# Attention stage of a one-core MoE kernel: q loaded in rows of six tokens, outputs computed in two row halves of the array

## What is computed

```
kv = np.einsum('bhsd,bhse->bhde', k, v)
out = np.einsum('bhsd,bhde->bhse', q, kv)
rms = np.sqrt(np.mean(out * out, axis=-1, keepdims=True) + 1e-06)
return (out / rms * g_norm).astype(np.float32)
```

## Time and profile before

| | |
|---|---|
| median of 3 runs | 1157.27 us (1157.14 to 1159.4) |
| the profiled execution, its own time | 1156.55 us |
| its span | 1155.0 us |
| PE busy | 1127.1 us, 98% of the span |
| DVE, ACT, POOL busy | 732.2, 454.6, 657.8 us |
| attention stage on PE | to 72.37 us |

### The profile page before, as it was taken

How to read it: one execution, slowest core, us unless ns; L and a number is a source line. 1 busy time by engine, 2 the same in 40 slices (tenths; PEclk the granted TensorE clock), 3 DMA queues, 4 the chain that set the end, 5 groups by cost and what they waited for, 6 DMA issues and landing times.

```text
span 1155.0 us, 18656 instructions
## 1 busy us (share of the span) xinstructions
PE 1127.1 (98%) x6184; PEld 993.1 (86%) x6185; DVE 732.2 (63%) x1160; ACT 454.6 (39%) x807; POOL 657.8 (57%) x609
## 2 busy tenths in 40 slices
PE   8989999999999999999999999999999999999996
PEld 7878999988989888988989888988987888888885
DVE  3876888888875878888875878888662222222221
ACT  4774444444534444444534444444322222222220
POOL 1477777799867777799867768777330111111101
PEclk8999999999999999999999999999989999999998
DMA  9936877777712348777712348777379849427960
GB/s 236 248 88 207 283 281 273 278 258 267 254 37 73 113 154 299 273 263 266 256 37 73 112 156 300 271 260 279 137 265 355 308 182 360 162 93 300 364 252 13
DMA packets 102434, 250.87 MB, mean 217 GB/s; under 512 B 8255, under 2 KB 48191, under 8 KB 94172
## 3 DMA queue, kind: packets, MB, share of 16 engines
q1 hardware_dynamic: 97360, 235.18, 59.3%
q0 software_dynamic: 4800, 14.72, 3.6%
q10 hardware_dynamic: 203, 0.05, 0.0%
HBM read 170.99 MB, written 79.98 MB: 217 GB/s over the span
## 4 chain that ended last, share of the span: by engine, by line
PE 85%; DVE 6%; POOL 3%; issue 2%; DMA 2%; ACT 1%; SPq 0%; DVEq 0%; POOLq 0%; ACTq 0%
PE ps L1257 27%; PE ps L1259 26%; PE ps L1258 26%; PE ps L1446 2%; PE ps L1350 1%; PE ps L1214 1%; PE ps L1412 1%; DVE hT_lo L941 1%; DVE x_rows L952 1%; DMA w_raw<-in_moe_w_dram 1%; DVE hT_lo L934 1%; PE ps L1335 1%; DMA q<-in_q_dram 1%; DVE hT_lo L939 1%; POOL x_ops_lo L515 1%
## 5 line engine op out<-in xcount | busy, mean ns | idle before, releaser
L1257 PE MATMUL ps<-x_ops_hi,w_hi 128*128 128x384 f32 x672 | 226.9, 338 | 4.1 <-DVE sum L922 4.0
L1257 PE MATMUL ps<-w_hi,hT_hi 128*128 128x512 f32 x576 | 227.3, 395 | 1.8 <-DVE x_rows L952 1.5
L1259 PE MATMUL ps<-x_ops_hi,w_lo 128*128 128x384 f32 x672 | 225.8, 336 | 0.0
L1259 PE MATMUL ps<-w_hi,hT_lo 128*128 128x512 f32 x576 | 225.3, 391 | 0.0
L1258 PE MATMUL ps<-w_lo,hT_hi 128*128 128x512 f32 x576 | 225.1, 391 | 0.0
L1258 PE MATMUL ps<-x_ops_lo,w_hi 128*128 128x384 f32 x672 | 225.0, 335 | 0.0
L952 DVE SCALAR_TENSOR_TENSOR x_rows<-ps,dense_probs,x_rows 128x512 f32<-128x512 f32 x270 | 190.2, 738 | 22.9 <-PE ps L1259 22.9
L607 POOL DMA_INDIRECT out_dram<-y_rows,row_ids x22 | 22.6, 1027 | 236.2 <-DVE y_rows L1155 141.8
L491 POOL TENSOR_TENSOR w_lo<-w_raw,w_hi 128x512 fp32r<-128x512 f32 x96 | 148.4, 1566 | 8.0 <-ACT w_hi L694 8.0
L1145 DVE TENSOR_TENSOR rhT_lo<-ps,rhT_hi 128x512 fp32r<-128x512 f32 x44 | 28.4, 686 | 172.0 <-ACT rhT_hi L813 172.0
L477 POOL TENSOR_TENSOR w_lo<-w_raw,w_hi 128x512 fp32r<-128x512 f32 x48 | 62.3, 1299 | 129.9 <-ACT w_hi L684 129.9
(11 more groups left out here) (198 smaller groups left out, 2013.3 us busy)
## 6 DMA issues: line engine op xcount, KB each, us to landing
w_slots<-split_parts SPq DMA_DIRECT2D x64, 1024.0 KB, 5.8
w_raw<-in_moe_w_dram SPq DMA_DIRECT2D x96, 512.0 KB, 3.6
ahead_raw<-in_moe_w_dram SPq DMA_DIRECT2D x64, 512.0 KB, 6.7
split_parts<-ahead_hi SPq DMA_DIRECT2D x64, 512.0 KB, 3.9
split_parts<-ahead_lo SPq DMA_DIRECT2D x64, 512.0 KB, 5.7
row_tile<-dispatched_rows POOLq DMA_DIRECT2D x20, 257.0 KB, 5.4
kv<-in_k_dram SPq DMA_DIRECT2D x16, 288.0 KB, 8.0
kv<-in_v_dram SPq DMA_DIRECT2D x16, 288.0 KB, 8.9
```

What stands on the lines that cost most here:

```text
L1257: mm(out_, ah, bh, start=(first and m == 0), stop=False, skip_group_check=not final or not first)
L1259: last = mm(out_, al, bh, start=False, stop=(final and m == n - 1), skip_group_check=not final or not first)
```

## The change

- q is loaded by one DMA per unit, laid out as k and v are: six following tokens on a partition, runs of 6 x 64 floats. The six transposes stay six; each now takes tokens 2j and 2j+1 of the six.
- `kv_blocks` holds for each head the 64x64 block once on partitions 0 to 63 and once on 64 to 127, 64 columns wide, with no zeros. ACT writes it alone: one copy of 128x64 for the halves that stay where they are, and two of 64x64 for those that cross. `copy_kv` on DVE and the zeroing on POOL go.
- `outputs(u)` has 12 matmuls rather than six: even tokens with weights and data on rows 0 to 63, odd tokens on rows 64 to 127, 64 columns moving, the two going to two PSUM banks (`out_banks`).
- PE runs 8 filler matmuls at the start of `products_in(1)` and 3 between its k-v products and its transposes.
- The x parts on ACT are made in turns 5, 7, 10, 11, 12, 13, 14 rather than 5, 7, 10, 11, 11, 12, 12.

```diff
-    QG = S // (2 * NP_)
+    QG = SJ // 2
...
-    qs = [at(f"q{s}", [NP_, QG, 2, 2 * DH], F32, (o if s < 2 else kvq23) + 9216 * (s % 2) + 6144) for s in range(KVS)]
+    qs = [at(f"q{s}", [NP_, 2, KHD], F32, (o if s < 2 else kvq23) + 9216 * (s % 2) + 6144) for s in range(KVS)]
...
-                for h in range(2):
-                    sp.dma_start(qs[s][:, :, h, :], q_h[u, h]).then_inc(q_in[s], 16)
+                sp.dma_start(qs[s][:, :, :], q_u[u]).then_inc(q_in[s], 16)
...
-            g.memset(kvb[:, :, :, :], 0.0).then_inc(consts_made, 1)
...
                 A(qT[:, s, :, :], qT_banks, ACT.Copy).then_inc(in_copied, 1)
+                A(kvb[:, s, 0, :], psf[:, KV0:KV0 + DH], ACT.Copy).then_inc(in_copied, 1)
                 for h in range(2):
-                    hp = slice(h * DH, (h + 1) * DH)
-                    A(kvb[hp, s, h, hp], psf[hp, KV0:KV0 + DH], ACT.Copy).then_inc(in_copied, 1)
+                    A(kvb[(1 - h) * DH:(2 - h) * DH, s, 1, :], psf[h * DH:(h + 1) * DH, KV0:KV0 + DH], ACT.Copy).then_inc(in_copied, 1)
...
-                for i, at_ in zip(X_ORDER, (5, 7, 10, 11, 11, 12, 12)):
+                for i, at_ in zip(X_ORDER, (5, 7, 10, 11, 12, 13, 14)):
...
-            def copy_kv(u, s):
-
-                dve.wait_ge(in_copied, 3 * u + 3)
-                if u == 0:
-                    dve.wait_ge(consts_made, 1)
-                for h in range(2):
-                    hp, other = slice(h * DH, (h + 1) * DH), slice((1 - h) * DH, (2 - h) * DH)
-                    V.tensor_copy(kvb[other, s, h, other], psf[hp, KV0:KV0 + DH]).then_inc(kv_copied, 1)
...
+            def fillers(n):
+                for _ in range(n):
+                    mm(ps[:, 7, 0:P], ident[:, :], ident[:, :], start=True, stop=True)
+
             def products_in(u, s, n_in):
 
+                if u == 1:
+                    fillers(2 * WARM // 3)
                 if u:
-                    pe.wait_ge(in_copied, 3 * u)
-                    pe.wait_ge(kv_copied, 2 * u)
+                    pe.wait_ge(in_copied, 4 * u)
...
+                if u == 1:
+                    fillers(WARM // 4)
+                pe.wait_ge(q_in[s], n_in // 2)
...
-                        to = out_bank[s][:, j * 2 * P:(j + 1) * 2 * P].rearrange("p (t h d) -> p t h d", t=2, h=2)[:, :, h, :]
-                        last = mm(to, qT[:, s, h, j * NP_:(j + 1) * NP_], kvb[:, s, h, :].rearrange("m (t d) -> m t d", t=2), start=True, stop=True)
+                        for t in range(2):
+                            tp = slice(t * DH, (t + 1) * DH)
+                            last = mm(out_banks[s][:, t, (2 * j + h) * DH:(2 * j + h + 1) * DH], qT[tp, s, h, j * NP_:(j + 1) * NP_],
+                                      kvb[tp, s, h if t == 0 else 1 - h, :], start=True, stop=True)
```

More of the change, by code:

```diff
@@ L113, in build @@
     qT = at("qT", [P, 2, 2, QH], F32, o2)
-    kvb = at("kv_blocks", [P, 2, 2, P], F32, o2 + 4608)
-    sq = at("squares", [NP_, QW], F32, o2 + 6656)
+    kvb = at("kv_blocks", [P, 2, 2, DH], F32, o2 + 4608)
+    sq = at("squares", [NP_, 2, QW // 2], F32, o2 + 6656)
     hsum = at("head_sums", [NP_, 3, 4 * QG], F32, o2 + 9728)
@@ L242, in seq @@
                 "u two (p j) d -> u p two (j d)", p=NP_)
-        k_u, v_u = seq(k), seq(v)
-        q_h = q.rearrange("b (u two) s d -> (b u) two s d", two=2).rearrange("u two (g p t) d -> u two p g (t d)", t=2, p=NP_)
+        q_u, k_u, v_u = seq(q), seq(k), seq(v)
         w1a_u = w1a.rearrange("e (c p) (f n) -> e f p c n", p=P, n=FQ)
@@ L252, in build @@
         qT_banks = psf[:, 0:1024].rearrange("m (h n) -> m h n", h=2)[:, :, 0:QH]
-        out_bank = [psf[0:NP_, (2 + 2 * s) * 512:(2 + 2 * s) * 512 + QW] for s in range(2)]
-        xT_bank = psf[:, 6 * 512:6 * 512 + QW].rearrange("m (g t p) -> m g p t", t=2, p=P)[:, :, 0:NP_, :]
+        out_banks = [ps[0:NP_, 2 + 2 * s:4 + 2 * s, 0:QW // 2] for s in range(2)]
+        xT_bank = psf[:, 6 * 512:6 * 512 + QW].rearrange("m (j p) -> m j p", p=P)[:, :, 0:NP_].rearrange("m j (g p) -> m g p j", g=SPB)
         KV0 = 512 + 320
@@ L449, in _ @@
             g.memset(fill[:, :], 0.0).then_inc(consts_made, 1)
-            pool.wait_ge(consts_made, 7)
+            pool.wait_ge(consts_made, 6)
             pool.wait_ge(powers_made, 2)
@@ L655, in square @@
                 act.wait_ge(o_done, u + 1)
-                A(sq[:, :], out_bank[s], ACT.Square).then_inc(o_squared, 1)
+                A(sq[:, :, :], out_banks[s], ACT.Square).then_inc(o_squared, 1)
             def root(u):
@@ L967, in _ @@
             dve.wait_ge(p_step, 7)
-            dve.wait_ge(consts_made, 14)
+            dve.wait_ge(consts_made, 13)
             steps = [0]
@@ L1223, in transposed @@
                     pe.wait_ge(x_out, u)
-                for j in range(2 * QG):
-                    last = tr(psf[:, 6 * 512 + j * P:6 * 512 + j * P + NP_], yn[:, s, j * P:(j + 1) * P], ident[0:NP_, 0:NP_])
+                for t in range(2):
+                    for j in range(QG):
+                        to, of = 6 * 512 + (2 * j + t) * P, (t * QG + j) * P
+                        last = tr(psf[:, to:to + NP_], yn[:, s, of:of + P], ident[0:NP_, 0:NP_])
                 last.then_inc(xT_done, 1)
-            pe.wait_ge(consts_made, 3)
-            for _ in range(WARM):
-                mm(ps[:, 7, 0:P], ident[:, :], ident[:, :], start=True, stop=True)
+            pe.wait_ge(consts_made, 2)
+            fillers(WARM)
             products_in(0, 0, 32)
```

25 lines of the change are left out of this document (10 added, 15 removed).

## The result

The changed kernel takes 1183.55 us (median of 4 runs, 1180.21 to 1184.87), the kernel before 1157.2 (1156.11 to 1159.4) beside it on the same chip: a ratio of 1.023, with a 95% interval of 1.0213 to 1.0247. The forecast was 1149.3, with 1154.7 as the high end. The profiled execution took 1183.71, its span is 1182.0 against 1155.0.

What follows compares the result with a forecast made beforehand. PE, busy 98% of the span, bounds the kernel; in attention the loop and loads are near-bounds. Terms -5.0 - 2.2 - 0.3 - 0.5 = -8.0 against 1156.55, with the median 0.7 above that execution: 1149.3 us, range 1147.5 to 1154.7.

Steps and rivals of the forecast that it cites:

- Rival 1: Attention loop: the clock falls to 1.2 GHz, 2.2 us per unit; half the units gives 1162 us; chance 8%.
- rival 3: Ramp: the clock falls there all the same, -3 in place of -5.0, 1151.3 us; chance 12%.
- The ramp, -5.0: Start of attention stage: fillers keep the clock up, so outputs 3 start at 22.35 rather than 27.37.
- Outputs, 0.87 us: A unit's 24 row-half output records take 0.87 us rather than 1.40; bounds 0.80 and 1.78.
- rival 4: Outputs: weight loads of the row halves run alone, outputs 1.78 us, 1158.3 us in all; chance 9%.
- The loop, 6.66: Two-unit attention loop: 7.03 + 0.16 (ACT) - 0.53 (outputs) = 6.66 us; six loops give -2.2.
- X parts, -0.3: Twelve units of the loop: spreading ACT's doubled x parts over turns saves 0.3 us (0 to 0.7).
- the end, -0.5: Outputs 15, ahead of the dense stage, are 0.53 us shorter.
- The pace of 2.8: Attention-stage loads: q's longer rows bring a unit's loads from 3.51 to 2.8 us, no longer a bound.
- Rival 2: Attention-stage loads keep their pace of 3.5 us a unit; gain at most 2.7, 1154.6 us; chance 9%.
- unit 4 there near 19: End of ramp: loads at 2.8 us a unit bring unit 4 near 19 us; it is needed at 19.5.
- a dense stage that hands the gain back: Sign of being wrong: the dense stage's first steps wait for POOL and hand the 8 us back.

Runs made afterwards that it cites:

- the kernel with fillers in units 6 to 8: Changed kernel plus three whole-array filler matmuls ahead of the outputs of units 6, 7 and 8 only: 1166.65 and 1168.78 us.
- the whole-array kernel: Changed kernel's q load, fillers and moved x parts, but outputs, kv_blocks and copies as in the kernel before: 1156.73 us, ratio 1.000.
- the changed kernel with 128 columns: Changed kernel with each row-half output matmul reading its 64 columns twice, so 128 stream: 1158.82 us, ratio 1.0032.
- one filler: Changed kernel plus one whole-array filler ahead of every unit's outputs: two executions at 1157.23 and 1159.12 us, seven from 1184.29 to 1192.03, one at 1170.07.
- the kernel with fillers in units 0 to 5: Changed kernel plus three whole-array filler matmuls ahead of the outputs of units 0 to 5 and none after: 1165.78 us.

## Why the prediction was wrong, step by step

**The step that failed** is the one that left the clock full in the loop. Rival 1 named the mechanism, with 8% and, for its price, half of the units. It held in all of them, after a fall in the ramp (rival 3's condition). The argument against it, PE busy for 1.70 of 3 us at clock 1.00, was taken from a loop whose outputs stream 128 columns, and I carried it over to a loop of 64-column records. The change had altered just what the row's evidence rested on. Nor did I ask the two questions apart: what lets a full clock fall, and what brings a fallen one back. In the kernel before, the fall in the ramp cost 10 us of half clock because the loop with outputs of 128 columns restored it; with 64 a like fall costs the whole stage.

**Its price.** 2 x 2.76 = 5.5 us for a unit at 1.2 GHz was nearly right: 5.70. What was mis-sized is how long it lasts: 2.2 for each of twelve units is 26.4, and with the -8.0 that makes 1175.7. Counted on the traces, the forecast's first dense matmul at 64.37 became 96.51: 5.45 of the 32.1 between are the ramp (27.80 for 22.35), 25.3 the twelve units (66.60 for 41.27) and 1.4 the end (2.11 for 0.73). The half clock at the start of the dense stage costs some 2 more, which makes 34.1 of the 34.25 from 1149.3 to 1183.55.

**The ramp, -5.0.** Measured +0.43. Its first part held: fillers under other waits, clock 1.00 to 15.08, outputs 0 at 13.17 (forecast 12.85; a wait of 0.58 for probs_rows had been left out). Rival 3, the clock falling in the ramp all the same, thus happened, but was priced on the loop's recovering from it. The term was too large even with the clock held: the kernel with fillers in units 6 to 8 runs the changed kernel's own program up to unit 5, and in its execution the clock stayed full to 27.06. Its outputs 3 start at 23.91, 3.5 us earlier than before. Of the missing 1.5, 1.1 is outputs 0 at 13.92 for 12.85, and the rest the three units.

**Outputs, 0.87 us.** 1.16 at full clock in the changed kernel itself (13.17 to 14.33), 1.17 in others. Within the bounds of 0.80 and 1.78, and the halves do overlap (rival 4 is out). The size was off because I took a pair of 96-column weight loads for the k-v pair's 72 ns: it is 1.17 / 12 = 97, where k-v pairs with 64 weight columns have 0.85 / 12 = 71. The Trainium skill, page TensorE: Matmul & The Clock Gate, section LDWEIGHTS, has a weight load go by its columns at 1.2 a nanosecond; 80 ns for 96 and 53 for 64 differ by 27, and the measured pairs by 26. I had set the rule aside for the transposes' row, and for sizes between two widths it was the better guide.

**The loop, 6.66.** 6.94 where the clock was held. ACT's +0.16 was +0.06 (1.73 for 1.83), the outputs' -0.53 was -0.23, and a third term, put at nothing, is +0.10: row-half outputs start 0.62 us behind the transposes ahead of them (58.42 to 59.04 in the kernel with fillers in units 6 to 8), where it was 0.52 (33.88 to 34.40 in the earlier trace rows). The three make it 6.96. So -0.5 for six loops rather than -2.2.

**X parts, -0.3, and the end, -0.5.** The first was not measured apart; the whole-array kernel, with the spread x parts and a full clock, takes 44.45 for the twelve units where it was 43.77, so no gain is seen (an "issue" pause of 1.12 us is in it). The end was +0.88 at half clock; at full clock 1.40 to 1.17 would be -0.2. PE waited for nothing of POOL at the start of the dense stage.

**Loads.** SP's long waits came as forecast. The pace of 2.8 didn't: 3.2 to 3.35. At half clock that cost nothing. Where the clock held it did, right behind the ramp: PE waits for the k-v load of unit 5 for 1.65 us with fillers in units 6 to 8 and for 1.55 in the changed kernel with 128 columns (27.09). Rival 2 was the better guess on the pace, and the forecast's "unit 4 there near 19" left no room for it. Later in the stage nothing waits for loads.

**Had the clock held,** the terms as measured would be -3.5, -0.5 and -0.2, but the wait for the load takes back part of the first at once. The k-v products of unit 5 start at 26.80 in the kernel with fillers in units 6 to 8, and in the kernel before here:

```profile
28.78 0.92 PE L1199 MATMUL ps<-kv 96*64 96x64 f32 x24
```

That is 2.0 us, so some 2.7 in all at the first dense matmul, an estimate from these rows. In the whole-array kernel 2.1 there became a ratio of 1.000 (0.9987 to 1.0014) at the end. The forecast named a dense stage that hands the gain back among what would make it wrong, without a price. Nor do the chances of its list add up to the 0.80 for faster: 0.58, 0.12 and half of 0.09 are 0.75. So no version run here beats the kernel before; those that hold the clock end 0.0 to 0.4% from it.

**Open.** What tips the clock isn't settled. Of the nine traced executions with fillers in unit 1, two lost it near 15 us: those with the longest wait for probs_rows near 12 us, 0.58 (the changed kernel) and 0.82 (one filler). The seven others waited for 0 to 0.51 there and held it past that point; 0.50 is that of the kernel with fillers in units 6 to 8, whose program is the same up to unit 5. That sorts the traces, and a load that comes a little sooner or later may be why one program holds the clock in some executions and loses it in others, but no run has varied this wait alone. Later, pauses of 1.3 to 2.2 us stood ahead of the falls in loops of 64-column records, while one of 1.55 did nothing in the changed kernel with 128 columns, nor did this one in the kernel before (clock 1.00 in 69 to 72):

```profile
70.62 0.69 PE L1225 MATMUL ps<-ident,attn_rows 96*128 96x96 f32 x6 [1.30 <-DVE x_raw L880]
```

Two of these pauses are "issue", in which PE waited for nothing that the profile names. The longest, in the kernel with fillers in units 0 to 5, and its DMA queue of instructions from 46 to 55 us:

```profile
51.13 0.45 PE L1189 MATMUL ps<-kv 96*64 96x64 f32 x8 [2.22 <-issue]
```

```profile
q8 instruction: 1, 0.02, 0.9%
```

That one packet has 16 KB, from 48.51 to 49.78, while PE stands from 48.91 on. Each of the four "issue" pauses over 0.7 us in these traces ends 1.3 to 1.7 us behind such a packet (35.59 behind 33.94, 51.93 behind 50.22, 35.58 behind 33.99), and the packets come further apart where PE is slower: 8 to 9 us in the kernel before from 41 us on, 12 to 14 in the changed kernel from 43 on. So PE may have waited for its own instructions, with the queues full of loads; that isn't tested.

## What to carry to other kernels

When a change makes matmuls smaller, the clock at which they run is part of its price: a row that shows PE at full clock at a low busy share speaks only for the matmuls in that row, and "busy 100%" at clock 0.50 may be a state that the loop never leaves. Ask separately what the new loop does with a full clock and what it does with a fallen one, and look for pauses ahead of a fall (0.58 to 2.2 us here). A gain in a stage is a gain only if what the next stage waits for (here the load of w_raw and POOL's sums) comes earlier too, and if the loads can follow: here outputs 3 came 3.5 us sooner and the next k-v products, which waited for their load, only 2.0.

## What the hardware showed that I had not expected

- PE was busy for 80.5 of the 81 us from 15 to 96 in the changed kernel, and its clock stayed at 1.2 GHz for 85 us; with PE busy for all of 116 us it did so in the one with whole-array outputs in 24 records of 64 columns. The Trainium skill, page TensorE: Matmul & The Clock Gate, Part 1, puts the fall down to idle gaps and the return to being busy; here it returned or not by the form of the outputs, at PE busy 8.70 of 8.70 and 11.40 of 11.40 us. The trace of the changed kernel disagrees: PE is busy, and the clock doesn't return.
- In loops of 64-column records full clock was lost behind pauses of PE of only 1.3 to 2.2 us, and near 15 us with no pause but 0.58 and 0.82 at 12.
- At 1.2 GHz, 24 whole-array records of 64 columns take 4.00 us, and 12 of 128 columns 2.88: the same columns in all, yet 39% more time. Each record brings a load of 96 weight columns.
- 24 records of 128 columns on row halves take 1.48 us at full clock (34.12 to 35.60), 12 on the whole array 1.40: streams in the two halves overlap nearly fully.
